# At most two index scatters under way: POOL waits for the second last one before it issues the next

## What is computed

```python
# attention over keys and values that are averaged in groups of 8 (8 batches, 8 heads, 576 rows, 64 wide)
k_p = k.reshape(B, H, Sp, pool, D).mean(axis=3); v_p = v.reshape(B, H, Sp, pool, D).mean(axis=3)
attn = softmax(np.matmul(q, k_p.transpose(0, 1, 3, 2)) / sqrt(D))
x = np.matmul(attn, v_p)                      # laid out as 4608 tokens x 512
# mixture of experts: each token goes to the best 2 of 8 experts (512 -> 1024 -> 512)
noisy = x @ w_gate + log1p(exp(x @ w_noise)) * noise
top2, top2_w = best two of noisy, their softmax
out[token] = sum over its two experts: weight * (relu(x @ w1[e]) @ w2[e])
# a last layer over all tokens (512 -> 2048 -> 512)
h = out @ w_in;  y = (h - tanh(h)) @ w_out
```

## Time and profile before

| | |
|---|---|
| three runs | 2034.49, 2035.42 (median), 2036.87 us |
| profiled execution | 2034.7 us, of it the span of the core 2032.7 us |
| PE busy | 1918.5 us, 94% |
| DVE, ACT, POOL busy | 1000.0, 820.3, 531.1 us |
| index scatters L497 | 96, 89.1 us, 928 ns on average |

### The profile page before, as it was taken

One profiled execution on the slowest core, in us unless ns is written; L12 is line 12 of the kernel. 1 busy time (PEld: TensorE's weight loads), 2 busy tenths in 40 slices (PEclk: granted clock), 3 DMA queues, 4 the chain that ended last, 5 costly groups with the idle time before them and its releaser, 6 DMA issues.

```text
span 2032.7 us, 36169 instructions
## 1 busy us (share of the span) xinstructions
PE 1918.5 (94%) x13072; PEld 1747.2 (86%) x13073; DVE 1000.0 (49%) x1928; ACT 820.3 (40%) x1720; POOL 531.1 (26%) x532
## 2 busy tenths in 40 slices
PE   5888867999999999999999979999999999999999
PEld 5787767889899999999998968999988999998898
DVE  3767563332322313131323227677777667777765
ACT  4766651332322323231323224444444444444444
POOL 2244433221221112111221222222322223322222
PEclk9978778999999999999999989999999999999999
DMA  8766531332321314131322230110000011000000
GB/s 207 169 131 137 116 104 57 135 114 73 104 78 45 124 41 134 52 124 41 114 72 93 82 108 27 58 36 31 31 31 31 31 48 45 31 31 31 31 31 21
DMA packets 107721, 152.41 MB, mean 75 GB/s; under 512 B 50624, under 2 KB 75328, under 8 KB 104864
## 3 DMA queue, kind: packets, MB, share of 16 engines
q1 hardware_dynamic: 81600, 98.98, 15.9%
q0 software_dynamic: 26080, 52.90, 9.7%
HBM read 111.52 MB, written 40.33 MB: 75 GB/s over the span
## 4 chain that ended last, share of the span: by engine, by line
PE 84%; DVE 5%; issue 4%; another core or an unknown queue 3%; ACT 2%; DMA 1%; DVEq 0%; POOL 0%; ACTq 0%; POOLq 0%; SPq 0%
PE banks L767 13%; PE banks L766 13%; PE banks L765 13%; PE banks L758 13%; PE banks L756 13%; PE banks L757 13%; PE banks L746 3%; PE banks L633 1%; ACT pr L912 1%; PE banks L654 1%; DVE mx L1142 1%; DMA k_raw<-in_k 1%; DVE x_sb L1152 1%; PE banks L642 0%
## 5 line engine op out<-in xcount | busy, mean ns | idle before, releaser
L756 PE MATMUL banks<-x_hi,w_hi 128*128 128x256 f32 x2304 | 640.4, 278 | 9.7 <-DVE x_lo L1316 6.1
L758 PE MATMUL banks<-x_hi,w_lo 128*128 128x256 f32 x2304 | 640.3, 278 | 4.3 <-issue 4.2
L757 PE MATMUL banks<-x_lo,w_hi 128*128 128x256 f32 x2304 | 640.1, 278 | 4.2 <-issue 4.0
L765 PE MATMUL banks<-w_hi,h_hi 128*128 128x512 f32 x1184 | 467.2, 395 | 3.0 <-DVE h_lo L1398 3.0
L767 PE MATMUL banks<-w_hi,h_lo 128*128 128x512 f32 x1184 | 465.9, 394 | 0.0
L766 PE MATMUL banks<-w_lo,h_hi 128*128 128x512 f32 x1184 | 463.0, 391 | 0.0
L756 PEld LDWEIGHTS banks<-x_hi,w_hi 128*128 128x128 f32 x2304 | 436.4, 189 | 13.6 <-DVE x_lo L1316 7.1
L757 PEld LDWEIGHTS banks<-x_lo,w_hi 128*128 128x128 f32 x2304 | 436.1, 189 | 7.9 <-issue 5.4
L758 PEld LDWEIGHTS banks<-x_hi,w_lo 128*128 128x128 f32 x2304 | 436.3, 189 | 4.0 <-issue 4.0
L596 POOL TENSOR_SCALAR large<-u_sq 128x512 uint8<-128x512 f32 x144 | 222.4, 1545 | 585.4 <-ACT u_sq L1071 317.8
L1323 DVE SCALAR_TENSOR_TENSOR h_lo<-banks,h_hi 128x512 fp32r<-128x512 f32 x144 | 99.6, 692 | 380.7 <-ACT h_hi L1000 193.3
(11 more groups left out here) (156 smaller groups left out, 2123.9 us busy)
## 6 DMA issues: line engine op xcount, KB each, us to landing
w_raw<-in_moe_w SPq DMA_DIRECT2D x32, 1024.0 KB
y<-y_rows SPq DMA_DIRECT2D x18, 1024.0 KB, 5.0
q_sb<-in_q SPq DMA_DIRECT2D x32, 288.0 KB, 4.7
x_rows<-x_sb SPq DMA_DIRECT2D x64, 144.0 KB, 2.7
out_x<-y_sb SPq DMA_DIRECT2D x36, 256.0 KB, 2.1
k_raw<-in_k SPq DMA_DIRECT2D x16, 288.0 KB, 3.4
v_raw<-in_v SPq DMA_DIRECT2D x16, 288.0 KB
k_raw<-in_k POOLq DMA_DIRECT2D x16, 288.0 KB, 4.6
```

Of the source, the lines that this page charges most:

```text
L756: pe.matmul(part, hi, x_hi[:, c, :], start=(c == 0), stop=False)
L757: pe.matmul(part, hi, x_lo[:, c, :], start=False, stop=False)
L758: mm = pe.matmul(part, lo, x_hi[:, c, :], start=False, stop=(c == NC - 1))
L765: pe.matmul(p_y[m][:, :], hi, w_hi[par][:, o:o + DM], start=(j == 0), stop=False)
```

## The change

`scattered` becomes two semaphores. The scatters use them in turn. Ahead of each scatter from the third of a batch on, POOL waits until the second last one has landed. In the loop the value of that wait depends on the batch, so it is worked out in a register. Everyone who waited for `scattered` now waits for both semaphores at half the count.

```diff
-        r_step, routed, scattered, route_out = ... sem("scattered"), ...
+        scattered = [sem(f"scattered{i}") for i in range(2)]
...
             sp.wait_ge(counted, 1)
-            sp.wait_ge(scattered, 16 * 2 * TT * B)
+            for i in range(2):
+                sp.wait_ge(scattered[i], 16 * TT * B)
...
                 for i in choices:
                     for t in range(TT):
+                        n = i * TT + t
+                        if n >= 2:
+                            pool.wait_ge(scattered[n % 2], b * 16 * TT + 16 * (n // 2))
+                            settle(pool)
                         pool.indirect_dma_start(slot_row, ...slot_i[:, i, t:t + 1]...,
-                                                ...row_id...).then_inc(scattered, 16)
+                                                ...row_id...).then_inc(scattered[n % 2], 16)
...
-                wait(dve, scattered, b * 16 * 2 * TT)
+                for i in range(2):
+                    wait(dve, scattered[i], b * 16 * TT)
```

More of the change, by code:

```diff
@@ L215, in attention_moe_ffn @@
         diff_ready, ed_ready, m_ready, pos_done = sem("diff_ready"), sem("ed_ready"), sem("m_ready"), sem("pos_done")
-        r_step, routed, scattered, route_out = sem("r_step"), sem("routed"), sem("scattered"), sem("route_out")
+        r_step, routed, route_out = sem("r_step"), sem("routed"), sem("route_out")
+        scattered = [sem(f"scattered{i}") for i in range(2)]
         settled = sem("settled")
@@ L496, in scatter @@
                     for t in range(TT):
+                        n = i * TT + t
+                        if n >= 2:
+                            pool.wait_ge(scattered[n % 2], b * 16 * TT + 16 * (n // 2))
+                            settle(pool)
                         pool.indirect_dma_start(slot_row, bass.IndirectOffsetOnAxis(ap=slot_i[:, i, t:t + 1], axis=0),
-                                                row_id[:, i * TT + t:i * TT + t + 1], None).then_inc(scattered, 16)
+                                                row_id[:, i * TT + t:i * TT + t + 1], None).then_inc(scattered[n % 2], 16)
             add_values(0, 0)
@@ L520, in _ @@
                 body(b)
-            pool.wait_ge(scattered, 16 * 2 * TT * (B - 3))
+            for i in range(2):
+                pool.wait_ge(scattered[i], 16 * TT * (B - 3))
             pool.dma_start(rows_a[:, :], slot_row.rearrange("(p n) o -> p (n o)", n=COLS)[:, 0:AHEAD * SUB]).then_inc(rows_a_in, 16)
@@ L547, in _ @@
             send(0, rows_a, 0)
-            pool.wait_ge(scattered, 16 * 2 * TT * B)
+            for i in range(2):
+                pool.wait_ge(scattered[i], 16 * TT * B)
             for p in range(PAIRS):
```

## The result

| kernel | time, us (median, lowest to highest, runs) | profiled execution |
|---|---|---|
| before | 2034.95 (2033.45 to 2036.87, 4) | span 2032.7 |
| after | 1999.24 (1997.22 to 2003.62, 4) | 2000.64, span 1999.1 |

The ratio is 0.9827, with a 95% interval of 0.9807 to 0.9847. The forecast was 2041 us, so the change went the other way by 36 us; 1999 is the neighbourhood of rival B's half (1998).

A forecast was written before the change was run, and what follows sets the result against it. PE was taken as the bound, with 74 us of stalls beside scatters. First halves +3.5, second halves -5 and runs of twelve +6.8 made +5.3 us, so 2041 us on the 2035.4 median; range 1990 to 2067, the sum's own 2022 to 2052.

The forecast's parts named there:

- rival B: POOL's queue depth or gapless scatters hold PE up, and the cap ends it: 1961 us, half 1998; chance 0.25.
- What bounds the kernel: PE waits without a named source beside POOL's scatters, 64 us, plus 10 us of issue pieces: 74 us.
- the rule for what the stall does with a pause: PE beside scatters: a stall lasts about its run's length less 1.0 us; recovery in a pause was assumed.
- the first halves' +3.5: Five first runs of six in the loop: each ends 0.7 us later, stall too, +3.5 us (0 to +7.5).
- the second halves' -5: Five second runs of six, cut in two by a pause: -1.0 us each, -5 us (-18.5 to +21).
- the twelves' +6.8: Three runs of twelve: +1.9 us each, 5.7, plus 1.1 for a later send: +6.8 us (0 to +13).
- Hardly more than two are under way: POOL's scatters before the change: one lands in 2.33 us, two take 2.43, so the cap hardly bites.
- 2.8 us per pair: Distance from scatter n-2 to scatter n under the cap: 2.8 us (2.43 to 3.21), instead of 2.43.
- The pause behind the adding DMA of v: Second halves: the ninth scatter waits for the seventh, queued behind v's 7.1 us; a pause of about 4 us.
- `y_sent` later: Last run of twelve: counted only about 343 us, ACT's copies move there, the send ends later, +1.1 us.
- A: Second halves: the stall lasts to the last landing despite the pause, +4.2 us each, 2067 us; chance 0.22.
- C: Everywhere, also behind v: the waits are already met when reached and do nothing, 2035 us; chance 0.13.

The follow-up runs named there:

- e17: Kernel before with memset pauses behind the second and fourth scatter of each half, no added wait for a scatter; stalled session, 2002.28 us (0.9844).
- e18: The change with three semaphores in turn, so three scatters may be under way; stalled session, 2014.31 us, ratio 0.9909 to before.
- e15: The change with four semaphores in turn, so four scatters may be under way; stalled session, 2028.69 us, ratio 0.9976 to before.
- e9: The change with its waits only in the three runs of twelve, the loop as before; stalled session, 2015.62 us, ratio 0.9921 to before.
- e6: The kernel after, unchanged, run again in a session where before has no stalls; 1995.55 us, ratio 1.0159 to before.
- e10: Kernel before with two tiny memsets behind each scatter; scatters wait until the second last is issued, not landed; stalled session, 2038.22 us (1.0027).
- e5: The kernel before, unchanged, run again in a session where it shows no stalls; 1963.22 us.
- e7: The change with one semaphore, each scatter waiting for the one ahead of it; session without stalls, 2123.42 us, ratio 1.0805 to before.

## Why the prediction was wrong

**What bounds the kernel: right in place, incomplete in price.** The unnamed pieces beside the scatters are what before has too much: 64 + 10 = 74 us by the chain, 71 us between the kinds of session. Not seen: a part of what a stall costs is clock after it (0.85 against 1.00 in a turn, 27.93 against 23.84 us of busy PE), and that they are not there in every session.

**The step that failed is the rule for what the stall does with a pause.** I took a stall as long as its run less 1.0 us, a function of the run's length, and so had longer runs cost more. A run that is drawn out stalls less, not more: e17 shows it with pauses alone, e18 and e15 in the dose. Whether that is the pace itself or the smaller number under way at once is open. With the rule fall the terms that stood on it, the first halves' +3.5, the second halves' -5 and 5.7 of the twelves' +6.8. Measured: the twelves -17 (e9), the loop about -19 by difference (both kinds of halves). The sum's own range was also added up wrongly: its bounds give about 2017 to 2051, not 2022 to 2052.

**"Hardly more than two are under way": mis-sized.** It rested on one landing of 2.33 us after the last scatter of a batch. Under the loop's traffic a scatter takes longer: in after, POOL's third scatter of a half came 3.0 to 4.7 us after the second, in first halves too, and 26 waits took 62.1 us, where my 2.8 us per pair had made some 0.4 each. In the runs of twelve many pairs came 2.84 us apart, as forecast (the rows below), but others up to 7.3 us, and the runs took 18.2 to 20.4 us from first to last start, where before took 13.4 and I had expected 15.3:

```profile
257.17 0.91 POOL L503 DMA_INDIRECT slot_row<-row_id,slot_i  x1 [3.14 <-DMA slot_row<-row_id,slot_i]
...
260.01 0.91 POOL L503 DMA_INDIRECT slot_row<-row_id,slot_i  x1 [0.72 <-issue]
...
262.87 1.03 POOL L503 DMA_INDIRECT slot_row<-row_id,slot_i  x1 [0.73 <-issue]
```

The price of the waits follows from this: 32 us (e6), where I had +5.3 with everything in it. POOL became the bound, and behind it DVE, which may write `row_id` only when the last scatter has landed (17.8 us of idle time), a wait that was met at once before.

**The pause behind the adding DMA of v: right in place, and in more places than I saw.** It is there, 3.2 to 3.7 us of idle time in the second halves (forecast 3 to 4), as the measured 7.1 us of v had it. The first halves of the later turns have it as well, 2.6 to 3.4 us. Before, POOL waited 15.64 us for the routing ahead of a first half, and v had landed by then; after, it waits 0.3 to 1.2 us there, so the first scatters stand right behind the adding DMA of v, as in the turn at 150.19, where that DMA started at 147.67. In the one first half that still has the long wait, at 91.99, the pause is 2.03 us. This reading rests on the order of the starts; no run tests it alone. By the fit of the Trainium skill's page "DMA: Bandwidth & Descriptors", section "Anatomy of one DMA — SWDGE (gpsimd) path", the data of v would be down after an estimated 2.7 us. The trace of before has 7.1 us, so here the fit is far too short.

**`y_sent` later: right in kind, mis-sized.** The whole end came earlier than before, the last scatter at 317.46, not 341.70. But ACT's copy waited 18.3 us for `y_sent`, to 317.35, and ACT could not turn to its next work, `h_hi`, until then. DVE waited 15.4 us for that (the longest of three such waits), and PE stood idle for 5.46 us. e9 has the same wait, and its trace names the chain to PE. DVE's wait and PE's in after, then PE's in e9:

```profile
DVE h_lo L1332 <- ACT h_hi L1042: 20.4, 3, 15.4
319.77 0.79 PE L773 MATMUL banks<-w_hi,h_hi 128*128 128x512 f32 x1 [5.46 <-issue]
```

```profile
335.51 0.80 PE L773 MATMUL banks<-w_hi,h_hi 128*128 128x512 f32 x1 [5.49 <-DVE h_lo L1332]
```

I had looked at the send alone, not at what stands behind the copy on ACT, and put +1.1 us on it. The granted clock was 0.80 in the ten microseconds from 320 us on, so some of this was paid twice, too. Also, rows 11 name PE as what released the copy at 336.86: they show that `y_sent` had been counted by then, so at least four DMAs ahead, and not that it was counted at that moment.

**The rivals.** A: wrong, of the unnamed pieces only the 3.40 us were left. C: wrong. B had the sign and the size. Of its two causes, the depth of the queue is ruled out (e10); scatters that follow with no gap fits all runs, with the number under way beside it as said above. My two arguments against it were the 2.33 us above, and a single piece of the chain at 341.46 us that began as the queue was emptying, which says nothing of the spacing. B's price for the half, 1998, hit for another reason than half a relief: nearly all of the relief, less 32 us of waits.

**Open.** What in a stalled session makes the engines stand: the trace shows DVE, ACT and PE waiting for releases without a source, and at the DMA engines nothing that would explain it (a share of 0.70 in one stall, 0.02 in another). Nor do I know what sets the kind of a session.

## What to carry to other kernels

When a profile shows idle time without a source beside a burst of small DMAs, space the burst before reasoning about its length, and try it with dummy work first: it tells whether a wait for the landing is needed. A cap on transfers under way costs its landing time under load, which has to be read beside the same traffic and not from a quiet stretch; here that was 32 us for two, 13 for three, 6 for four. And time the kernel before in more than one session before tuning against a stall: this one was worth 71 us in some and nothing in others.

## Unexpected of the hardware

- The same kernel before takes 1963 to 1964 us in three sessions and 2032 to 2035 in four, with the same work (107721 DMA packets, 13072 matmuls) and, in the two that have a trace, the unnamed waits in the second kind alone.
- 24 DMAs of 96 rows of 4 bytes each, side by side in DRAM, cost 39 (direct) and 43 us (indirect) beside the weights' loads, with POOL waiting 22.9 us for a load of k that it waits 11.9 us for in e5; far apart they cost 9, in a stalled session.
- A wait for a landed scatter on POOL costs more than the 2.33 us of the earlier trace rows: with one under way (e7) starts lie about 2.8 us apart at best, and with two (after) a scatter starts 2.8 to 7.3 us after the second last one.
